# Where POOL's weight and key/query splits stand in a slot, and who takes the second layer's lo parts

## The reference

```python
# attention: q, k, v [4, 8, 576, 64]
scores = (1 / 8) * q @ k.T
kth = np.partition(scores, -32, axis=-1)[..., -32:-31]
scores = np.where(scores >= kth, scores, -1e9)
attn = exp(scores - max) / (sum + 1e-9)
x = (attn @ v) laid out as [2304, 512]
# first layer: w_in [512, 2048], w_out [2048, 512]
h = x @ w_in
g = np.where(h >= 1, h, np.where(h <= -1, 0, (h + 1) ** 2 / 4))
x = g @ w_out
# second layer, with weights of its own
h = np.maximum(x @ w_in, 0)
out = (h * h) @ w_out
```

## Time and profile before

| | us |
|---|---|
| median of 3 runs | 1286.64 |
| lowest, highest | 1285.8, 1288.35 |
| the profiled execution | 1287.39 |
| its span in the trace | 1285.6 |
| TensorE busy | 1194.8 (93%) |
| VectorE busy | 910.6 (71%) |
| ScalarE busy | 721.8 (56%) |
| POOL busy | 783.9 (61%) |

### The profile page before, as it was taken

The page is one execution under the profiler, slowest core; times in us unless marked ns, Lnnn a source line. Parts: engine busy times, 40 slices in busy tenths (PEclk is TensorE's granted clock), DMA queues, the critical chain, the costliest instruction groups (busy, mean ns, idle before and its releaser), DMA issues.

```text
span 1285.6 us, 24517 instructions
## 1 busy us (share of the span) xinstructions
PE 1194.8 (93%) x8760; PEld 1132.5 (88%) x8760; DVE 910.6 (71%) x2039; ACT 721.8 (56%) x1617; POOL 783.9 (61%) x637
## 2 busy tenths in 40 slices
PE   2677888999999999999999999999999999999998
PEld 1566878988888999999999999999989999999997
DVE  5789899989899998989999999989861111111121
ACT  4555566766655476776767654556543565643332
POOL 2999787787788776777766767666562222222222
PEclk9966799999999999999999999999999999999999
DMA  5899748565879972543437851445429500780000
GB/s 194 275 341 349 255 164 274 187 232 209 321 254 341 387 300 74 170 166 122 130 114 263 314 197 39 140 151 198 147 77 354 217 34 1 265 325 8 27 17 17
DMA packets 98728, 245.89 MB, mean 191 GB/s; under 512 B 7344, under 2 KB 48304, under 8 KB 86320
## 3 DMA queue, kind: packets, MB, share of 16 engines
q1 hardware_dynamic: 98608, 244.33, 53.7%
HBM read 167.23 MB, written 77.07 MB: 190 GB/s over the span
## 4 chain that ended last, share of the span: by engine, by line
PE 69%; POOL 11%; ACT 8%; DVE 5%; issue 4%; DMA 1%; SPq 0%; ACTq 0%; POOLq 0%
PE h_ps L581 21%; PE y_ps L602 14%; PE y_ps L596 12%; PE pv_ps L540 6%; PE score_ps L581 6%; POOL s_sb L1045 4%; PE tr_ps L513 4%; POOL prob L1050 3%; PE score_ps L478 3%; DVE top L860 2%; DVE rest L862 2%; ACT prob L699 1%; POOL kq_lo L1029 1%; POOL w_out L1037 1%; ACT s_sb L676 1%
## 5 line engine op out<-in xcount | busy, mean ns | idle before, releaser
L1063 POOL TENSOR_TENSOR g_lo<-g_sb,g_hi 128x256 fp32r<-128x256 f32 x288 | 217.2, 754 | 405.1 <-ACT g_hi L778 404.9
L581 PE MATMUL h_ps<-xt_hi,w_in 128*128 128x256 f32 x1880 | 391.3, 291 | 3.5 <-DVE xt_lo L908 2.0
L581 PEld LDWEIGHTS h_ps<-xt_hi,w_in 128*128 128x128 f32 x1880 | 309.6, 191 | 6.7 <-issue 3.0
L860 DVE MAX8 top<-rest 128x8 f32<-128x576 f32 x432 | 303.8, 744 | 0.0
L1045 POOL TENSOR_SCALAR s_sb<-s_sb,top 128x576 f32<-128x576 f32 x144 | 258.4, 1794 | 51.5 <-DVE top L860 50.6
L581 PE MATMUL h_ps<-xt_lo,w_in 128*128 128x256 f32 x940 | 266.2, 283 | 0.0
L596 PE MATMUL y_ps<-g_hi,w_out 128*128 128x256 f32 x1152 | 232.6, 285 | 0.4 <-POOL g_lo L1063 0.3
L778 ACT ACTIVATE g_hi<-g_sb 128x256 fp32r<-128x256 f32 x288 | 121.0, 420 | 184.7 <-DVE g_sb L917 68.8
L862 DVE MATCH_REPLACE8 rest<-top,rest 128x576 f32<-128x576 f32 x288 | 211.4, 741 | 0.0
L602 PE MATMUL y_ps<-w_out,g_hi 128*128 128x512 f32 x576 | 203.3, 394 | 0.3 <-POOL g_lo L1063 0.3
L596 PEld LDWEIGHTS y_ps<-g_hi,w_out 128*128 128x128 f32 x1152 | 190.4, 193 | 1.7 <-POOL g_lo L1063 0.5
(11 more groups left out here) (79 smaller groups left out, 1954.9 us busy)
## 6 DMA issues: line engine op xcount, KB each, us to landing
w_in<-w_scratch SPq DMA_DIRECT2D x32, 1024.0 KB, 6.7
w_out<-w_scratch SPq DMA_DIRECT2D x32, 1024.0 KB, 8.0
ks<-ks_scratch SPq DMA_DIRECT2D x47, 576.0 KB, 5.5
qs<-qs_scratch SPq DMA_DIRECT2D x78, 256.0 KB, 4.4
stage<-in_w_dram SPq DMA_DIRECT2D x32, 512.0 KB, 4.7
w_scratch<-w_in SPq DMA_DIRECT2D x16, 1024.0 KB, 6.8
w_scratch<-w_out SPq DMA_DIRECT2D x16, 1024.0 KB, 8.3
v_sb<-in_vv_dram SPq DMA_DIRECT2D x48, 325.0 KB, 5.5
```

Of the source, the lines that this page charges most:

```text
L581: last = pe.matmul(h_bank(k), wi[:, f // 2, w, m, cols], x[:, m, :], start=(m == 0 and n == 0), stop=(m == KT - 1 and n == 2))
L860: dve.max(best, src[:, :]).then_inc(rank_step, 1)
L1063: pool.tensor_tensor(g_lo[k % 2][:, :], g_sb[k % 2][:, :], g_hi[k % 2][:, :].bitcast(F32), ALU.subtract).then_inc(g_lo_done, 1)
```

## The change

Two things change. `by_vector` now holds for every fourth block of the second layer and no longer for every second: VectorE keeps the lo parts of blocks 19, 23, 27 and 31, and POOL gets those of 17, 21, 25 and 29 in addition to its eight. And POOL's slot is written in another order: the kq split and the first weight split stand between g lo of q and g lo of q+1; a second weight split stands behind g lo of q+1.

```diff
 def by_vector(i):
-    return i >= WBLOCKS and i % 2 == 1
+    return i >= WBLOCKS and i % 4 == 3
...
             def split_w(i):
-                if by_vector(i):
-                    return
                 pool.wait_ge(w_hi_done, i + 1)
...
                 lo_at(q)
-                lo_at(q + 1)
+                new = [i for i in range(2 * WBLOCKS) if W_SLOT[i] == n and not by_vector(i)]
                 if n in PREP_SLOT:
                     split_kq(PREP_SLOT.index(n))
-                for i in range(2 * WBLOCKS):
-                    if W_SLOT[i] == n:
-                        split_w(i)
+                for i in new[:1]:
+                    split_w(i)
+                lo_at(q + 1)
+                for i in new[1:]:
+                    split_w(i)
```

## The result

| | before | after |
|---|---|---|
| median, us | 1288.35 | 1298.88 |
| lowest, highest | 1285.8, 1289.47 | 1295.46, 1301.76 |
| the profiled execution | 1287.39 | 1295.46 |
| its span | 1285.6 | 1293.7 |

Five runs of each, side by side. The changed kernel takes 1.0083 times the time of before, 95% interval 1.0061 to 1.0105: 0.8% **slower**. The profiled execution of after is the fastest of its five, so its trace shows 8.1 us of the 10.5 us between the medians.

The account below looks back on a forecast made before the run. Early on, a slot's first mask was taken to bound the kernel, from 397 us mostly TensorE's own work. Slot terms of +10.3 and clock +1.8 gave +12.1 on 1287.39, so 1299.5, less 0.75 for the median: 1298.7 us; range 1279 to 1307.

Parts of the forecast that it names:

- What bounds it, and the price: Up to 397 us the first mask sets the pace; g under a POOL split ends 0.27 to 0.29 us behind it.
- The term of seven single slots: Slots 12, 13, 15, 17, 19, 32, 41: one POOL split, no VectorE split, g held up, +6.3 us together.
- The signs named: Profile after: g 2.0 to 2.4 us under splits, POOL's g hi waits below 405 us, masks released by `top`.
- Slots with a late g: Slots 10, 11, 38, 44, 47: g 1.8 to 2.4 us behind, loses less than POOL's lateness, -1.0 us together.
- slots 20, 24 and 27: Slots where POOL takes two weight splits: -0.2, -0.3 and +0.3 us, together -0.2.
- Slot 25: Counted with the single POOL splits: g begins behind the g lo part of q and is held up, +0.7 us.
- I cost SP at nothing: SP's block staging and stores: lo counts come earlier or within 1 us of before, so no cost; blocks staged ahead.
- Slots 22 and 23: Slot 22: VectorE's split gone, g first at the port, -1.2 us; slot 23: VectorE's split stays, g held, +1.45.
- Slot 30: POOL's split at 405.75, g at 405.83: POOL first costs +1.2 us, VectorE first gives -0.6; POOL first taken.
- The clock: Behind slot 21 TensorE's wait grows from 1.31 to about 2.5 us and its clock falls: +1.8; early slots 0.
- (1): Rival: g held up little or not at all, POOL's lateness goes everywhere, 14.5 us gained, 1272 us; chance 0.15.
- (2): Rival: VectorE reaches the port first in about half of the slots, -1.2 us, 1285.4 us; chance 0.20.

Follow-up runs that it names:

- the other three traces: The changed kernel itself, unchanged, profiled three more times as second, third and fourth trace: 1295.42, 1295.5 and 1297.07 us.
- the first experiment: The changed kernel, with POOL's moved splits also waiting until VectorE has ended the g of step q+1: 1283.27 us, ratio 0.9970 to before.
- the write-only operations: The changed kernel, with POOL's splits in slots with a g at q+1 replaced by memsets that only write, lo parts zero: 1275.01 us, single run.
- the order alone: The kernel before with only the new order of POOL's slot, VectorE keeping its old eight lo parts: 1299.77 us, ratio 1.0096.
- the share alone: The kernel before with only POOL's larger share of the second layer's lo parts, POOL's slot in the old order: 1291.73 us, ratio 1.0042.
- the version that beats both: Kernel before, splits moved ahead of g lo of q+1 behind a wait for g, only where VectorE has no weight split: 1279.18 us, ratio 0.9945.
- block 21 given to POOL: The version that beats both, with block 21's lo part (slot 22) also moved from VectorE to POOL: 1279.09 us, ratio 0.9937 to before.
- the halves: Slots and share of the version that beats both, no wait, each split halved around the g lo part of q+1: 1283.13 us, ratio 0.9965.

## Why the prediction was right, and where not

The mechanism was right, and the median (1298.88) is close to the forecast (1298.7) by luck. The forecast started from a median before of 1286.64, and beside the changed kernel before took 1288.35: the medians differ by 10.5 us, where 12.1 were forecast. For the profiled execution the forecast was 1299.5 and it took 1295.46, 4.0 us less; the table above splits that, and in the other three traces the sum of the steps was 8.0, 8.1 and 9.7 us.

- **What bounds it, and the price.** Right. The first mask sets the slot, and a g that begins under a split ends 0.27 to 0.29 us behind it in all 16 of the 22 slots in which it did so (2.24 to 2.52 us in slots 11 to 19). The wait of the first experiment and the write-only operations take the price away in two different ways. The term of seven single slots was forecast at 6.3 and measured 6.8. The signs named show it: POOL's wait for g hi shorter, the masks of slots 13, 15, 17, 32 and 41 released by `top`, 2.34 to 2.36 us late each. One sign was half wrong: VectorE's four weight splits took 1.20, 1.68, 1.20 and, in slot 28, 2.52 us, not 1.2 throughout. And the prediction's first example, the g at 410.28 of before, is not one with two tiles: line 923 reads the one tile `r_sb` as both inputs, and is held up all the same (2.19 us in slot 32 of after, 0.27 us behind the split).
- **Slots with a late g, slots 20, 24 and 27.** Signs right, each sum within 0.5 us. But most of the late g's -1.2 is slot 11, and that goes with the clock: its mean from the mask of slot 10 to that of 11 was 0.85 in before, and 1.00, 0.86, 0.83 and 0.91 in the four traces of after, where the step was -0.76, -0.03, -0.09 and -0.75. Without it the five slots give about -0.5 us, half of the forecast.
- **Slot 25: +0.7 forecast, -2.44 measured.** Two steps failed. The g was not held: it began 0.11 us ahead of POOL's g lo part (343.76 and 343.87), where I had read it behind. And "I cost SP at nothing" was wrong. In before ScalarE's hi part in slot 25 waited 1.96 us for a block that was not yet staged; SP stages it behind the stores of slot 23's blocks, which wait for their lo parts. SP and ScalarE in before:

```profile
317.43 0.44 SPq L372 DMA_DIRECT2D w_scratch<-w_out  x1
...
336.47 1.06 ACT L669 ACTIVATE w_out<-stage 128x1024 fp32r<-128x1024 f32 x1 [1.96 <-DMA stage<-in_w_dram]
```

  and in after, where the second has no wait:

```profile
321.88 0.53 SPq L372 DMA_DIRECT2D w_scratch<-w_out  x1
...
341.44 1.05 ACT L669 ACTIVATE w_out<-stage 128x1024 fp32r<-128x1024 f32 x1
```

  The mask of slot 23 starts at 314.85 in before and at 322.35 in after, so the store was issued 2.6 us behind it and is now issued 0.5 us ahead of it. The experiments split by just this: where slot 23's split is moved (after, the wait, the order alone, the writes) the store is about 0.5 us ahead and ScalarE waits 0.22 us with the writes and not at all in the others; where it is not (before, the share alone, the version that beats both) the store is 2.3 to 2.6 us behind and ScalarE waits 1.96, 1.12 and 2.68 us. I had seen the 2 us and named them as a cover that might break; they were a loss in before that the earlier lo parts take away.
- **Slots 22 and 23: -1.2 and +1.45 forecast, -1.58 and +1.27 measured where the clock held.** The sum is near, the reason for slot 23 was not. Its g is not under the split at all (split to 315.26, g at 316.70). What was won in slot 22 is given back, because TensorE is not ready; ScalarE in the second trace:

```profile
307.77 0.38 ACT L766 ACTIVATE r_sb<-h_ps 128x256 f32<-128x256 f32 x1 [1.18 <-PE h_ps L581]
```

  The same pair stands in kernels in which nothing is held in these slots: -1.58 and +1.27 with the writes, -1.56 and +1.25 with block 21 given to POOL. I had put TensorE's limit at 1.2 us into slot 22, where it shows one slot later and takes back nearly all.
- **Slot 30: +1.2 forecast, -1.53 measured**, the wrong choice between two ends I had both named. I let the two engines keep the distance of before (POOL's split at 405.75, the g at 405.83). In after the g began 0.60 us behind POOL's g lo part and ahead of the split:

```profile
412.59 0.75 POOL L1061 TENSOR_TENSOR g_lo<-g_sb,g_hi 128x256 fp32r<-128x256 f32 x1
413.19 0.44 DVE L923 TENSOR_TENSOR g_sb<-r_sb 128x256 f32<-128x256 f32 x1 [0.62 <-ACT r_sb L764]
413.29 3.01 POOL L1029 TENSOR_TENSOR kq_lo<-kq_lo,kq_hi 128x1216 fp32r<-128x1216 f32 x1
```

  With the order alone POOL was first in the same slot (g 2.20 us, step +1.50). The distance of 0.79 us in before did not carry over, and less than 0.2 us of it decides.
- **Slot 26: +0.9 forecast, +2.13 measured.** The hi parts were not ready, though I had said they would be in all slots but 10 and 11: the split waited 0.81 us for ScalarE, so it ended later and held the g longer. POOL and VectorE in after:

```profile
357.32 2.38 POOL L1035 TENSOR_TENSOR w_out<-stage,w_out 128x1024 fp32r<-128x1024 f32 x1 [0.81 <-ACT w_out L669]
...
358.21 1.78 DVE L923 TENSOR_TENSOR g_sb<-r_sb 128x256 f32<-128x256 f32 x1 [2.40 <-ACT r_sb L764]
```

- **Slot 28: +1.2** lies between its two cases, +0.66 and +2.02.
- **The clock: +1.8 forecast**, 1.2 measured in the first trace, none in two others, so a term that held in two of four executions. Its place was right: the wait ahead went to 2.28 us. In the early slots I had taken it as 0. TensorE's waits went to 2.31 to 2.57 there, and in the first trace the clock fell behind one of them, but not behind another of the same 2.57 us:

```profile
215.00:225.00 10.00, 10.00 (x74) 9.97 (x73) 9.05 (x23) 5.24 (x14) 6.33 (x6) 0.83 0.93 333
```

  It fell in that stretch in all four traces of this kernel, down to 0.50, and the step of slot 16, which holds it, was +0.51, +0.17, +0.12 and +0.69, against +0.14 to +0.16 in the kernels with moved splits whose clock stayed there. In the third trace it also fell behind slot 13's wait (2.58 us), and slot 14 lost 0.98 us instead of 0.14. So the price of an early fall was between nothing and 0.8 us.
- **The slots I left at nothing** brought +2.5, most of it in 16, 18, 31 and 51. Slots 16 and 51 are the clock, as above. Slot 31's +0.50 stands in every kernel in which slot 30 gained 1.3 us or more and is -0.21 where it did not (the order alone, the halves): it takes back part of that gain. Slot 18's +0.75 is +0.95 to +0.97 where g is not held (the wait, the writes); I have no cause for it.
- **The rivals.** (1) is about what the kernel does when the port is free (1275.01), so its sum was sound and its condition wrong. (2) wanted VectorE first in half of the slots; it was in 5 of 22 (22, 25, 27, 28, 30), and in the other three traces not in 28; in the fourth not in 22 either.

## What to carry to other kernels

Idle time of one engine is not free if its work there shares a port with an engine that is on the path: before moving work into a gap, ask what the other engine issues during that gap, and give the whole rest of the moved operation as its price. If the gap is still wanted, put a wait for the other engine's short operation ahead of the long one (1.05 us of POOL's time here, for 2.1 us of VectorE's), and leave out the slots in which the later start meets another such operation. Where the order at the port hangs on a few tenths of a microsecond (0.01 us in slot 28, 0.35 in slot 22), forecast both orders with a chance each, since single executions of one kernel go both ways.

## What the runs showed of the hardware

- POOL operations that only write SBUF do not hold up VectorE's two-input operation: 0.42 us under writes, 2.51 under a reading split of the same place.
- Starts recorded 0.01 us apart do not tell who gets the port: VectorE's record is the earlier one in both traces of slot 28, and it took 0.43 us in one (POOL 3.10) and 3.10 us in the other.
- How far behind POOL the g ends depends on POOL's operation: 0.27 to 0.29 us behind the end of a split, a g lo part or a mask multiply, but 0.70 to 0.72 us ahead of the recorded end of a mask compare (1.73 us), in all 45 places of before where a g took over 0.55 us under one.
- When VectorE's g begins while POOL's short g lo part still runs, it is served ahead of POOL's next queued split (slots 22 and 30 of after: 0.47 and 0.44 us, the split then 2.60 and 3.01 us instead of 2.38 and 2.81).
- The same wait of TensorE (2.28 us, at the same place of the program) was followed by a clock of 0.50 in two executions and of 1.00 in two others.
- The clock's fall reaches other engines: a later h made g miss its place at the port and cost 2.3 us in slot 22 (fourth trace) and 1.0 us in slot 51 (first), more than the 1.2 us and the 0.2 to 0.3 us that the fall cost there where g kept it.
